# Two slots of raw input weights, another order at the transition, and EPS as a row of the values

## The reference, cut to what matters

```python
mask = np.abs(pos[:, None] - pos[None, :]) < factor
scores = np.where(mask, scale * q @ k.T, -1e9)
attn = np.exp(scores - scores.max(-1)); attn /= attn.sum(-1) + 1e-9
out = np.repeat(out_pooled, factor, axis=2) + attn @ v
x = (sigmoid(x @ w_gate) * (x @ w_val)) @ w_out          # 512 -> 1536 -> 512
h = x @ w_in; y = (h * sigmoid(1.702 * h)) @ w_out2      # 512 -> 2048 -> 512
```

## Time and profile before

| | |
|---|---|
| median of 3 runs | 909.59 us (908.54 to 912.97) |
| profiled execution: time, span | 909.52 us, 907.7 us |
| mean granted clock of TensorE | 0.996 |
| busy: PE / DVE / ACT / POOL | 892.2 / 517.4 / 481.9 / 694.1 us |
| all queues | 79.59 MB, mean 88 GB/s |

### The profile page before, as it was taken

The page is one execution under the profiler, slowest core; times in us unless marked ns, Lnnn a source line. Parts: engine busy times, 40 slices in busy tenths (PEclk is TensorE's granted clock), DMA queues, the critical chain, the costliest instruction groups (busy, mean ns, idle before and its releaser), DMA issues.

```text
span 907.7 us, 17629 instructions
## 1 busy us (share of the span) xinstructions
PE 892.2 (98%) x6566; PEld 833.1 (92%) x6566; DVE 517.4 (57%) x975; ACT 481.9 (53%) x964; POOL 694.1 (76%) x547
## 2 busy tenths in 40 slices
PE   8989999999999999999999999999999999999998
PEld 6777789999999999998989999999999898988987
DVE  5767645555555555566565555555665656565565
ACT  5767655454445455455555455554555554544542
POOL 5768689999779999778787679998777877565641
PEclk9999999999999999999999999999999999999999
DMA  9856122222222222211212122422222121232111
GB/s 320 242 176 192 49 70 70 71 70 70 70 71 70 70 71 70 71 70 47 94 47 81 59 70 70 140 71 70 70 70 70 52 88 47 93 117 74 67 47 70
DMA packets 26516, 79.59 MB, mean 88 GB/s; under 512 B 3136, under 2 KB 3136, under 8 KB 26432
## 3 DMA queue, kind: packets, MB, share of 16 engines
q1 hardware_dynamic: 26432, 78.48, 26.3%
HBM read 73.75 MB, written 4.72 MB: 86 GB/s over the span
## 4 chain that ended last, share of the span: by engine, by line
PE 94%; POOL 2%; DVE 2%; issue 1%; ACT 1%; ACTq 0%; POOLq 0%
PE o_ps L402 39%; PE d_ps L414 7%; PE d_ps L412 7%; PE d_ps L415 7%; PE s_ps L412 6%; PE s_ps L414 6%; PE s_ps L415 6%; PE t_ps L414 3%; PE t_ps L415 3%; PE t_ps L412 3%; PE o_ps L375 1%; PE o_ps L395 1%; DVE o_tok L1019 1%; PE d_ps L327 1%; PE t_ps L387 1%
## 5 line engine op out<-in xcount | busy, mean ns | idle before, releaser
L1147 DVE TENSOR_TENSOR att<-o_ps,att 128x512 f32<-128x512 f32 (+1 forms) x246 | 153.0, 625 | 150.6 <-PE o_ps L402 150.6
L1339 POOL TENSOR_TENSOR w_lo<-w_sum,w_hi 128x1024 fp32r<-128x1024 f32 x60 | 144.2, 2404 | 65.0 <-ACT w_hi L708 65.0
L1334 POOL TENSOR_TENSOR w_lo<-w_raw,w_hi 128x768 fp32r<-128x768 f32 x60 | 110.8, 1847 | 29.2 <-ACT w_hi L704 29.2
L414 PE MATMUL d_ps<-xs_lo,w_hi 128*128 128x384 f32 x360 | 120.9, 336 | 0.0
L412 PE MATMUL d_ps<-xs_hi,w_hi 128*128 128x384 f32 x360 | 120.7, 335 | 0.0
L415 PE MATMUL d_ps<-xs_hi,w_lo 128*128 128x384 f32 x360 | 120.7, 335 | 0.0
L1350 POOL TENSOR_TENSOR v_lo<-v_raw,v_hi 128x1024 fp32r<-128x1024 f32 x42 | 100.9, 2403 | 24.5 <-ACT v_hi L712 24.5
L1314 POOL TENSOR_TENSOR w_sum<-w_raw 128x256 f32<-128x256 f32 x120 | 88.5, 738 | 37.0 <-PE t_ps L415 28.7
L402 PE MATMUL o_ps<-v_hi,g_lo 128*128 128x512 f32 x288 | 114.0, 396 | 0.0
L402 PE MATMUL o_ps<-v_lo,g_hi 128*128 128x512 f32 x288 | 113.6, 394 | 0.0
L402 PE MATMUL o_ps<-v_hi,g_hi 128*128 128x512 f32 x288 | 111.9, 389 | 0.0
(11 more groups left out here) (120 smaller groups left out, 2053.8 us busy)
## 6 DMA issues: line engine op xcount, KB each, us to landing
v_raw<-in_w_out_dram SPq DMA_DIRECT2D x42, 512.0 KB, 3.5
w_raw<-in_w_gate_val_dram SPq DMA_DIRECT2D x36, 512.0 KB, 3.4
w_raw<-in_w_in_dram SPq DMA_DIRECT2D x24, 512.0 KB, 3.5
vw<-in_v_win_dram SPq DMA_DIRECT2D x32, 170.6 KB
vt<-in_v_tok_dram SPq DMA_DIRECT2D x16, 320.0 KB, 4.4
qk<-in_q_t_dram SPq DMA_DIRECT2D x16, 288.0 KB, 4.1
qk<-in_k_t_dram SPq DMA_DIRECT2D x16, 288.0 KB, 5.0
out_dram<-att SPq DMA_DIRECT2D x18, 256.0 KB, 4.3
```

Of the source, the lines that this page charges most:

```text
L414: pe.matmul(bank, wh[:, w, cols], xl[:, x, c, :], start=False, stop=False, skip_group_check=True)
L1147: vec.tensor_tensor(part, value, part, ALU.add).then_inc(y_added, 1)
L1334: gp.tensor_tensor(w_lo[b % 2][:, A11:A22 + 1, :], w_raw[:, R11:R22 + 1, :], w_hi[b % 2][:, A11:A22 + 1, :], ALU.subtract).then_inc(wa_rea ...
L1339: gp.tensor_tensor(w_lo[b % 2][:, S1:S4 + 1, :], w_sum[b % 2][:, S1:S4 + 1, :], w_hi[b % 2][:, S1:S4 + 1, :], ALU.subtract).then_inc(ws_re ...
```

## The change

`w_raw` gets a second slot, so that block b+2 can be loaded when block b is done; block 1 is loaded at SP's turn 4 instead of 7, block 2 at turn 9 and the second output group at turn 10 instead of after the loop. GpSimd's four sums of a block become four steps (`sum_in_1` to `sum_in_4`), of which block 1 gets one in each of the turns 8 to 11; T3's low part moves from turn 14 to 13, and ACT rounds block 1 at turn 8. At the transition PE does p6(0) before `turn_pooled(last)` and `weigh(last)` before p5(0), with ACT and DVE in the same order; the table of the sigmoid is loaded one turn earlier. And the EPS is no longer added by DVE: the values of every window get a 57th row, zero but for EPS in the column of the sums, and `e` a 57th key that is always 1. `p_t` gets 64 columns a window, the last 16 of them ones, so that `weigh` writes all 64 rows and the maximum with 0.5 is not needed. L1012 goes. The core of the diff (indices `[b % 2]` of `w_raw` and renamed functions are left out):

```diff
-        w_raw = place("w_raw", [P, 4, WG])
+        w_raw = [place(f"w_raw{i}", [P, 4, WG]) for i in range(2)]
...
-        p_t = place("p_t", [P, NWIN, QW])
+        p_t = place("p_t", [P, NWIN, HK])
...
                 for h in range(2):
-                    sp.dma_start(vw[u % 2][HK * h:HK * h + KW].rearrange("p w d -> p (w d)"), v_win[u, KW * h:KW * (h + 1)]
+                    sp.dma_start(vw[u % 2][HK * h:HK * h + KW + 1].rearrange("p w d -> p (w d)"), v_win[u, (KW + 1) * h:(KW + 1) * (h + 1)]
                                  ).then_inc(vw_loaded[u % 2], 16)
...
-                if b >= 1:
-                    sp.wait_ge(wa_ready, b)
-                    sp.wait_ge(wsum_ready, b)
+                if b >= 2:
+                    sp.wait_ge(wa_ready, b - 1)
+                    sp.wait_ge(wsum_ready, b - 1)
...
-                if i == 7:
+                if i == 4:
                     load_in(1)
-            load_in(2)
-            load_out(1)
+                if i == 9:
+                    load_in(2)
+                if i == 10:
+                    load_out(1)
             load_in(3)
+            load_in(4)
...
-                    load_in(LAST[k + 1] + 1)
+                    load_in(LAST[k + 1] + 2)
                 if k + 2 < NG:
-                    load_in(FIRST[k + 2] + 1)
+                    load_in(FIRST[k + 2] + 2)
...
-                            rows = slice(HK * h, HK * h + KW)
-                            mm = pe.matmul(o_ps[HK * par:HK * par + QW, h, pair * VC:(pair + 1) * VC],
+                            rows = slice(HK * h, HK * h + KW + 1)
+                            mm = pe.matmul(o_ps[HK * par:HK * (par + 1), h, pair * VC:(pair + 1) * VC],
                                            p_t[rows, w, :], vw[u % 2][rows, w, :], start=True, stop=True)
...
             weigh_pooled(last - 1)
+            p6(0)
             turn_pooled(last)
-            p6(0)
+            weigh(last)
             pe.wait_ge(exped_d, UNITS)
             pe.wait_ge(v_summed, UNITS)
             p5(0)
-            weigh(last)
             p7(0)
...
+                if i == 8:
+                    round_in(1)
...
+                if i == last - 1:
+                    snap_p1(0)
+                    nc.scalar.activation(token[:, 1:2], token[:, 0:1], ACT.Sigmoid)
                 if i == last:
-                    round_in(1)
-                    snap_u2(0)
-                    nc.scalar.activation(token[:, 1:2], token[:, 0:1], ACT.Sigmoid)
+                    round_in_sums(1)
                     sig11(0)
                     snap_u3(0)
                 drain_pooled(i)
                 if i == last - 1:
-                    snap_p1(0)
+                    snap_u2(0)
...
-            round_in_sums(1)
             sig22(0)
...
-                vec.tensor_scalar(den[:, :].rearrange("p (h a) -> p h a", h=2), sums[:, :, :, D], EPS, 0.5, ALU.add, ALU.max
-                                  ).then_inc(den_ready, 1)
-                dve.wait_ge(den_ready, u + 1)
-                vec.reciprocal(inv[:, :], den[:, :]).then_inc(inv_ready, 1)
+                vec.reciprocal(inv[:, :].rearrange("p (h a) -> p h a", h=2), sums[:, :, :, D]).then_inc(inv_ready, 1)
...
-            vec.memset(e[:, :, :, KW:HK], 0.0)
+            vec.memset(e[:, :, :, KW:KW + 1], 1.0)
+            vec.memset(e[:, :, :, KW + 1:HK], 0.0)
...
-            vec.memset(o_ps[:, :, :], 0.0).then_inc(zeroed, 1)
+            vec.memset(p_t[:, :, QW:HK], 1.0).then_inc(zeroed, 1)
...
+            c11(0)
             add_levels(UNITS - 2)
-            c11(0)
...
                 if i == 8:
                     pool.wait_ge(added, KC + 2)
                     sum_t1(0)
-                    sums_in_begin(1)
+                    sum_in_1(1)
...
+                    sum_in_2(1)
...
+                    sum_in_3(1)
...
+                    sum_in_4(1)
...
                 if i == 13:
                     low_x_sum(0, T1, 5)
+                    low_x_sum(0, T3, 6)
                 if i == 14:
-                    low_x_sum(0, T3, 6)
                     low_x_sum(0, T4, 7)
             low_x(0, B22, quarter[1, 1], 3)
-            sums_in_end(1)
             low_in(1)
             low_in_sums(1)
-            low_in(2)
-            sums_in_begin(2)
-            sums_in_end(2)
-            low_in_sums(2)
+            split_in(2)
             low_out(0)
...
-    ins["v_win"] = pack(_np.stack([v_pad[:, :, QW * w:QW * w + KW] for w in range(NWIN)], 3).reshape(UNITS, 2 * KW, NWIN * VC))
+    v_end = _np.zeros((UNITS, 2, 1, VC), v.dtype)
+    v_end[:, :, :, D] = EPS
+    v_win = [_np.concatenate([v_pad[:, :, QW * w:QW * w + KW], v_end], 2) for w in range(NWIN)]
+    ins["v_win"] = pack(_np.stack(v_win, 3).reshape(UNITS, 2 * (KW + 1), NWIN * VC))
```

More of the change, by code:

```diff
@@ L135, in attention_mlp_kernel @@
         warm = place("warm", [P, 2 * P], BF16)
-        small = place("small", [P, 6 * PAIRS + 26])
-        nmax, den, inv = (small[:, 2 * PAIRS * i:2 * PAIRS * (i + 1)] for i in range(3))
-        nmax_d, bias_d, den_d0, den_d1, plus_d, inv_d = (small[:, 6 * PAIRS + 4 * i:6 * PAIRS + 4 * (i + 1)] for i in range(6))
+        small = place("small", [P, 4 * PAIRS + 26])
+        nmax, inv = (small[:, 2 * PAIRS * i:2 * PAIRS * (i + 1)] for i in range(2))
+        nmax_d, bias_d, den_d0, den_d1, plus_d, inv_d = (small[:, 4 * PAIRS + 4 * i:4 * PAIRS + 4 * (i + 1)] for i in range(6))
         den_d = [den_d0, den_d1]
-        token = small[:, 6 * PAIRS + 24:6 * PAIRS + 26]
+        token = small[:, 4 * PAIRS + 24:4 * PAIRS + 26]
         held = top[0]
@@ L182, in attention_mlp_kernel @@
         weighed = sem("weighed")
-        den_ready, inv_ready = sem("den_ready"), sem("inv_ready")
+        inv_ready = sem("inv_ready")
         normed, turned_o, added = sem("normed"), sem("turned_o"), sem("added")
@@ L230, in load_vw @@
                 for h in range(2):
[L231 removed]
+                    sp.dma_start(vw[u % 2][HK * h:HK * h + KW + 1].rearrange("p w d -> p (w d)"), v_win[u, (KW + 1) * h:(KW + 1) * (h + 1)]
                                  ).then_inc(vw_loaded[u % 2], 16)
             def load_in(b):
[L236 removed]
+                if b >= len(BLOCKS):
                     return
[L238 to L240 removed]
+                if b >= 2:
+                    sp.wait_ge(wa_ready, b - 1)
+                    sp.wait_ge(wsum_ready, b - 1)
                 k, m = BLOCKS[b]
                 q, lay, p, g = GROUPS[k]
[L243 to L244 removed]
+                sp.dma_start(w_raw[b % 2][:, :, :].rearrange("p a n -> p (a n)"), w_gate_val[g, m] if lay == 1 else w_in2[g]
+                             ).then_inc(w_loaded[b % 2], 16)
             def load_out(k):
@@ L682, in copy_turned @@
                 for b, pairs in enumerate((range(PT0), range(PT0, PAIRS))):
-                    c = nc.scalar.copy(p_t[:, 2 * pairs.start:2 * pairs.stop, :],
+                    c = nc.scalar.copy(p_t[:, 2 * pairs.start:2 * pairs.stop, 0:QW],
                                        t_ps[:, b, 0:len(pairs) * P].rearrange("p (w k) -> p w k", k=HK)[:, :, 0:QW])
@@ L699, in round_in @@
             def round_in(b):
-                act.wait_ge(w_loaded, 16 * b + 16)
+                act.wait_ge(w_loaded[b % 2], 16 * (b // 2) + 16)
                 if b >= 2:
                     act.wait_ge(in_done[b % 2], NP * (b // 2))
-                nc.scalar.copy(w_hi[b % 2][:, A11:A22 + 1, :], w_raw[:, R11:R22 + 1, :]).then_inc(wahi_ready, 1)
+                nc.scalar.copy(w_hi[b % 2][:, A11:A22 + 1, :], w_raw[b % 2][:, R11:R22 + 1, :]).then_inc(wahi_ready, 1)
             def round_in_sums(b):
@@ L1312, in sum_in, with sum_in_1, sum_in_2, sum_in_3 @@
             def sum_in(b, name, a, c, op):
[L1314 to L1319, removed]
+                return gp.tensor_tensor(w_sum[b % 2][:, name, :], a, c, op)
+            def sum_in_1(b):
+                pool.wait_ge(w_loaded[b % 2], 16 * (b // 2) + 16)
                 if b >= 2:
                     pool.wait_ge(in_done[b % 2], NP * (b // 2))
-                sum_in(b, S1, raw[:, R21, :], raw[:, R22, :], ALU.add).then_inc(wsum_step, 1)
+                sum_in(b, S1, w_raw[b % 2][:, R21, :], w_raw[b % 2][:, R22, :], ALU.add).then_inc(wsum_step, 1)
+            def sum_in_2(b):
                 pool.wait_ge(wsum_step, 2 * b + 1)
[L1324 to L1328, removed]
+                sum_in(b, S2, w_sum[b % 2][:, S1, :], w_raw[b % 2][:, R11, :], ALU.subtract).then_inc(wsum_step, 1)
+            def sum_in_3(b):
+                sum_in(b, S3, w_raw[b % 2][:, R11, :], w_raw[b % 2][:, R21, :], ALU.subtract)
+            def sum_in_4(b):
                 pool.wait_ge(wsum_step, 2 * b + 2)
-                sum_in(b, S4, raw[:, R12, :], into[:, S2, :], ALU.subtract).then_inc(wsum_ready, 1)
+                sum_in(b, S4, w_raw[b % 2][:, R12, :], w_sum[b % 2][:, S2, :], ALU.subtract).then_inc(wsum_ready, 1)
             def low_in(b):
                 pool.wait_ge(wahi_ready, b + 1)
```

(14 more changed lines are left out.)

2 lines of the change are left out of this document (1 added, 1 removed).

## The result

| | before | after |
|---|---|---|
| median | 910.45 us (908.54 to 912.97, 6 runs) | 935.67 us (933.31 to 936.20 but for one, 6 runs) |
| ratio | | 1.0271 [1.0249, 1.0292] |
| profiled execution: time, span | 909.52, 907.7 us | 936.2, 934.5 us |
| mean granted clock | 0.996 | 0.978 |

One execution of after took 5004 us and is left out of the ratio. The change costs 2.7%, 25 us; the forecast was 922.8, with 912 to 935 as its range. Direction and mechanism were right. The size was not: the forecast took too high a rate for a DMA engine and left out a piece of PE's own way.

A forecast was written before the change was run, and what follows sets the result against it. TensorE work, filling 98% of the span, bounded the kernel; three DMA engines would come to bound attention. 907.7 + 17.0 - 3.7 = 921.0 us of span, so 922.8 us; range 912 to 935.

The forecast's parts named there:

- The spread: Value transfers `vw`: 57 rows would use 3 engines in place of 14, giving 2784 small packets in place of 3136.
- Rival 1: Value transfers stay spread over 15 or 16 engines, or vary their three, and the gains stand: 903 to 908 us; chance 0.10.
- The rate of one engine: Attention part: 23.7 GB/s per DMA engine, 7.4 us a unit on the three engines, `weigh(13)` 17.0 us later.
- 2 us of start and 0.5 of landing: Queue ahead of `weigh(13)`: engines full from about 2 us on, and 0.5 us added for the values to land.
- Rival 2: The engines bind but are not always full, or exceed 25.5 GB/s: within 0.5% of before, needing 27 GB/s; chance 0.07.
- The end of the attention part: `weigh(14)` follows `weigh(13)` at the later of PE's period, 5.84 us, and the next transfers, 5.9 us: no further loss.
- the cover ahead of `weigh(15)`: `vw` 15 takes 5.0 us more, PE needs some 6.7 us before `weigh(15)`: a cover of 1.7 us.
- Part 3: Two `w_raw` slots and new order at the transition: the 1.98 us stall and half clock go, 3.7 us gained.
- Part 2: The tensor_scalar L1012 of `normalise` goes: `turn_out` starts 0.20 us earlier, 2.0 us in all, hidden by the transfer wait.
- The wide stationary: `weigh` with 64 columns in place of 48: at worst 0.30 us a unit, 4 us over 14 units; at best nothing.
- Rival 3: Instruction packets, 18 with 0.29 MB up to 117 us, share one of the three engines: 12 us more, 935; chance 0.10.
- Rival 4: PE's clock falls in the waits, costing 1.7 us in a unit; absorbed, up to 2 us in all; no chance given.

The follow-up runs named there:

- 63 gives 9: Kernel before with value transfers of 63 rows in place of 56, the added rows unused: 915.13 us, ratio 1.0063.
- one transfer of 128: Kernel after with both heads' values padded to 64 rows and brought by one transfer of 128 partitions: 905.95 us, ratio 0.9956.
- 57-row kernel: Kernel before with only a 57th row, read by no product, in each head's value transfer: 937.73 us, ratio 1.0313.
- 58 rows: Kernel before with value transfers of 58 rows in place of 56, the added rows unused: 963.55 us, ratio 1.0585.
- PE kept busy: Kernel after with 12 unused products on constants ahead of each wait for values, units 0 to 14: 934.33 us, ratio 1.0267.
- part 3 alone: Kernel before with only the two `w_raw` slots and the new order; values, EPS and `normalise` as before: 905.39 us, ratio 0.9946.
- 56 + 1 cut: Kernel after with each head's 57 rows brought by two transfers, of 56 rows and of one row: 904.4 us, ratio 0.9927.
- the row loaded once: Kernel after with 56-row transfers, the EPS row put into both slots once at the start: 905.86 us, ratio 0.9962.
- 1560-byte rows: Kernel after with each value transfer cut into two of six windows, same bytes in twice the rows: 936.39 us, ratio 1.0276.

## Why the prediction was right and wrong, point by point

**The spread: right.** 56 gives 14 engines, 57 gives 3, 58 gives 2, 63 gives 9, and one transfer of 128 gives 16; the small packets are 2784 as computed. The rule of the Trainium skill (DMA: Bandwidth & Descriptors, section "Why a DMA increments its semaphore by 16 and not by 1"), the largest k up to 16 that divides the row count, agrees with all five. Rival 1 falls. That both halves use the same three engines no view shows, but the packet records do. From 3 us to 126.6 us, outside of instruction packets, fewer than three packets of SP's queue are under way in 0.5% of the time and exactly three in 32%. And the six shares of `vw` 15 are in at 136.25, 136.34 and 136.56, then at 138.58, 138.69 and 138.93 us: the second half some 19 rows of 120 ns behind the first. The count of packets also bears out that these engines have hardly a pause.

**The rate of one engine: the step that failed.** I took the middle, 23.7 GB/s, of 21.9 (15 us of full queues) and 25.5 (2 us of them), because long runs of rows seemed like weight loads. The last completion event of `vw` 13 comes in after at 127.06 us. With the 2 us of start and 0.5 of landing of the forecast, 2,720,704 B in 124.6 us are 21.8 GB/s. In the 57-row kernel it is 2,655,168 B and 120.76 us, 22.5, and with two engines 23.5. So the bound that I had written down (932.0) was nearly the result. From unit 2 to 12 the values landed every 8.6 us (34.53 to 120.16), where my rate gives 8.0 with the weight loads. The 0.5 of landing was right: the last row of `vw` 14 ends at 132.01, its event comes at 132.44, and a waiting `weigh` starts 0.09 behind such an event. The term is worth 127.1 - 117.3 = 9.8 us.

That the 21.9 of the earlier trace rows came so close is in part luck, for an engine has no fixed rate here:

- It goes with what the others do. Up to the landing of `vw` 13 a row of `vw` took 134 ns in after when at most three packets were under way and 161 when fourteen or more were. With 58 rows 70% of them moved in the first state, in after 48%, which goes with the better rate of the two engines; no run isolates it.
- The three engines are not level. Of `vw` 13 the first had its share in at 121.4 us and the last at 127.06, where with 57 rows alone they were within 0.4 us of each other (120.38 to 120.76). `weigh` waits for the last. Why one falls behind is open.

Rival 2 needed 27 GB/s. The best stretch shows 26.0 with only `vw` moving, and the whole way 21.8, so it falls, though an engine does go faster while the others rest.

**PE's own way from `weigh(12)` to `weigh(13)`: a term left out.** I let `weigh(13)` start when its values land. They land at 127.06, and PE comes at 130.88 without a wait: 3.8 us more. PE needs 7.67 us from `weigh(12)` in the kernel before (92.63 to 100.30, a stop of 1.41 for issue in it) and 7.68 with 57 rows, longer than the usual period, while the values of 12 and 13 land only 5.7 us apart there (115.1 and 120.8). In after `weigh(12)` itself came 1.1 us behind its values (121.30 and 120.16), and the unit behind it ran 9.58 us, 7.1 of them at half clock, while the values took 6.9. I could have read the 7.67 from the timeline of before. Such stops are in every kernel here, before too, but for the one with PE kept busy, whose waits have no "issue" at all; what they wait for no view says. How they share the 3.8 us with the clock was not isolated. With PE kept busy, where the clock fell less and no stop came, `weigh(13)` was 1.9 us behind its values (130.38 and 128.50), and 1.4 of that are the 12 products added ahead of it. So that kernel can't show what the stops cost. Together: 17.0 + 9.8 + 3.8 = 30.6, measured 30.5.

**The end of the attention part: right.** `weigh(14)` follows 5.77 us behind (5.9 forecast), and the cover ahead of `weigh(15)` held: no wait at 143.48.

**Part 3: right to a tenth.** 3.7 forecast, 3.7 measured by the profiled executions (the medians of part 3 alone say 4.2), and the rest behind `weigh(14)` is 797.8 to 798.0 us in each of the eight kernels that hold part 3. The new waits cost nothing: at 142.89 `turn_pooled(last)` starts without one.

**Part 2: right that it is hidden, but its size was off.** I held "nearly all" of 0.20 us a unit for real where values come in time. It is 0.10, since the next in line, ACT's `p_t` for `weigh_pooled`, was only that far behind; I had named what is late next for part 3, and not here. The wide stationary cost 0.03 us where my bound was 0.30, so nine tenths of that bound did not come.

**Rival 3 falls.** From 3 us to 126.6 us the instruction packets of after are under way for 19.3 us. If they went through one of the three engines, only two other packets would be under way wherever the wide transfers rest. The wide transfers rest in 12.4 us of the 19.3; in 10.7 of them three other packets are under way, in 1.7 fewer. So about one part in seven falls on the three engines, an estimated 2.6 us and not 12. That the rival's 935 came out is luck.

**Rival 4: rightly put, with one reservation.** The clock fell (41 us at half clock, before 6.8), and the waits absorbed it: keeping PE busy gave 1.3 us, inside the two intervals. The reservation is the unit behind `weigh(12)`, where PE and not a transfer was last.

**What beats both.** The change is worth keeping without its 57-row transfers. The 56 + 1 cut runs at 904.4 us, the row loaded once at 905.9, part 3 alone at 905.4: all faster than before by 0.4 to 0.7%, most of it by part 3.

## What to carry to other kernels

Before changing the partition count of a transfer, factor it: the largest divisor up to 16 is the number of engines that work, and a count of 57 or 58 can cost 3 to 6% where 56 or 128 cost nothing; an odd row goes by a transfer of its own or is loaded once. A low mean DMA share doesn't clear the transfers: divide the small packets by the number of transfers. To price a queue that will be full, trust no short stretch: a row took longer here while many others moved, and the last engine to finish counts. Then ask what the engine that waits still has to do when its data has landed.

## What the runs showed of the hardware that I had not expected

- An engine's rate was not fixed. A row of 3120 bytes of `vw` took 134 ns in after with at most three packets under way and 161 with fourteen or more. Three engines alone started one every 120 ns each (26.0 GB/s, from 137.3 us to 138.1 us); over the whole way it was 21.8 GB/s. Sixteen full engines moved 17.9, 21.9 or 23.8 GB/s each from 5 to 20 us, with transfers of 63, 56 or 128 rows.
- It went nearly by bytes (1560-byte rows 78 ns, 3120-byte rows 140, from 45 to 100 us).
- The narrow engines held up the wide transfers too: from 5 to 20 us the core moved 272 GB/s in place of 351. In that time SP spent up to 3.74 us on the issue of one transfer of k, where 0.4 is usual.
- Issuing four transfers in place of two cost nothing: the kernel with the lowest median here (56 + 1, 904.4 us) is one of the two with the most issues.
- The same wait for a transfer is booked as "issue" in after (11.9 us) and as a DMA wait with PE kept busy (9.0 us), and under both names with 57 and with 58 rows. The completion events tell what it is.
